# A linear attention chained to two gated networks: each head's 64x64 state in two quarters of the TensorE array

## What is computed

```python
def _attn_ref(q, k, v):
    q_s = exp(q - max(q, axis=-1)); q_s = q_s / (sum(q_s, axis=-1) + 1e-09)
    k_s = exp(k - max(k, axis=2));  k_s = k_s / (sum(k_s, axis=2) + 1e-09)
    kv = np.einsum('bhsd,bhse->bhde', k_s, v)            # a 64 x 64 state for each head
    return np.einsum('bhsd,bhde->bhse', q_s, kv)
x = attn_out.transpose(0, 2, 1, 3).reshape(B * S, H * D)  # 4608 tokens x 512
h = x @ w_in; r = maximum(h, 0); x = (r * r) @ w_out      # 512 -> 2048 -> 512
xn = x / sqrt(mean(x * x) + 1e-06) * rms_g
g = xn @ w_gate; y = (g * sigmoid(g) * (xn @ w_val)) @ w_out2  # 512 -> 1536 -> 512
```

## Time and profile before

| what | us |
| --- | --- |
| median of 3 runs | 1665.97 |
| lowest and highest of them | 1665.57, 1666.49 |
| profiled execution | 1665.29 |
| its span, from the first instruction to the last | 1663.5 |
| PE busy in the span | 1643.8 |

### The profile page before, as it was taken

How to read it: one execution, slowest core, us unless ns; L and a number is a source line. 1 busy time by engine, 2 the same in 40 slices (tenths; PEclk the granted TensorE clock), 3 DMA queues, 4 the chain that set the end, 5 groups by cost and what they waited for, 6 DMA issues and landing times.

```text
span 1663.5 us, 27042 instructions
## 1 busy us (share of the span) xinstructions
PE 1643.8 (99%) x10246; PEld 1496.7 (90%) x10246; DVE 1156.9 (70%) x1749; ACT 616.7 (37%) x1056; POOL 595.7 (36%) x470
## 2 busy tenths in 40 slices
PE   7999999999999999999999999999999998999999
PEld 6999999999988888888888989988988988999999
DVE  6687667666667778888766565546556568877775
ACT  5544334433323333333333333333333344334332
POOL 3554324332002225432237644555555552000000
PEclk9999999999999999999999999999999999999999
DMA  7675545554552353344342323232331244434441
GB/s 262 201 242 182 176 157 191 182 170 145 202 176 89 120 173 120 119 123 125 118 142 70 109 88 134 70 134 75 108 102 63 99 143 163 145 121 149 153 137 54
DMA packets 151745, 230.10 MB, mean 138 GB/s; under 512 B 11840, under 2 KB 75840, under 8 KB 151616
## 3 DMA queue, kind: packets, MB, share of 16 engines
q1 hardware_dynamic: 151616, 228.38, 41.5%
HBM read 143.39 MB, written 84.93 MB: 137 GB/s over the span
## 4 chain that ended last, share of the span: by engine, by line
PE 93%; POOL 2%; DVE 2%; issue 1%; ACT 1%; DMA 0%; SPq 0%; DVEq 0%; POOLq 0%; ACTq 0%
PE bank L1819 16%; PE bank L1820 16%; PE bank L1821 16%; PE bank L1905 7%; PE bank L1906 7%; PE bank L1907 7%; PE bank L1995 5%; PE bank L1996 5%; PE bank L1997 5%; PE bank L1812 2%; PE bank L1792 1%; PE bank L1808 1%; PE bank L1840 1%; PE bank L1841 1%; PE bank L1842 1%
## 5 line engine op out<-in xcount | busy, mean ns | idle before, releaser
L1819 PE MATMUL bank<-TR,SW 128*128 128x512 f32 (+1 forms) x840 | 308.5, 367 | 0.3 <-DVE TR L1554 0.3
L1821 PE MATMUL bank<-TR,SW 128*128 128x512 f32 (+1 forms) x840 | 308.7, 368 | 0.0
L1820 PE MATMUL bank<-TR,SW 128*128 128x512 f32 (+1 forms) x840 | 308.6, 367 | 0.0
L1819 PE MATMUL bank<-TAR,SA 128*128 128x288 f32 x784 | 249.1, 318 | 0.1
L1820 PE MATMUL bank<-TAR,SA 128*128 128x288 f32 x784 | 231.2, 295 | 0.0
L1821 PE MATMUL bank<-TAR,SA 128*128 128x288 f32 x784 | 230.4, 294 | 0.0
L1905 PE MATMUL bank<-GH,W 128*128 128x512 f32 x576 | 224.2, 389 | 0.4 <-DVE GH L1459 0.4
L1906 PE MATMUL bank<-GH,W 128*128 128x512 f32 x576 | 224.2, 389 | 0.0
L1907 PE MATMUL bank<-GH,W 128*128 128x512 f32 x576 | 224.2, 389 | 0.0
L1145 ACT ACTIVATE GH<-g 128x512 fp32r<-128x512 f32 x144 | 91.1, 634 | 241.6 <-DVE g L1454 161.6
L1995 PE MATMUL bank<-SW,OA 128*128 128x256 f32 x630 | 179.0, 284 | 0.0
(11 more groups left out here) (176 smaller groups left out, 3309.4 us busy)
## 6 DMA issues: line engine op xcount, KB each, us to landing
h_scratch<-hb SPq DMA_DIRECT2D x128, 288.0 KB, 2.6
hst<-h_scratch SPq DMA_DIRECT2D x144, 256.0 KB, 2.7
araw<-a_scratch SPq DMA_DIRECT2D x18, 1536.0 KB, 6.8
a_scratch<-group SPq DMA_DIRECT2D x72, 256.0 KB, 2.0
xst<-xn_scratch SPq DMA_DIRECT2D x10, 1024.0 KB, 5.1
xn_scratch<-x SPq DMA_DIRECT2D x9, 1024.0 KB, 5.4
a_scratch<-group SPq DMA_DIRECT2D x48, 192.0 KB, 1.9
out<-ost SPq DMA_DIRECT2D x36, 256.0 KB, 2.1
```

Source lines behind the costliest of these rows:

```text
L1819: nc.tensor.matmul(ps[:, 0:w], w_hi[:, cc], x_hi[:, c], start=opens and c == 0, stop=False, skip_group_check=True)
L1820: nc.tensor.matmul(ps[:, 0:w], w_lo[:, cc], x_hi[:, c], start=False, stop=False, skip_group_check=True)
L1821: last = nc.tensor.matmul(ps[:, 0:w], w_hi[:, cc], x_lo[:, c], start=False, stop=c == 1, skip_group_check=True)
```

## The change

In batches 1 to 7 X0 and X1 no longer split the tokens but the heads. X0 is head 0 (rows 0 to 63 of the array), X1 is head 1 (rows 64 to 127). Each is two matmuls with the same 64x64 weights, one diagonal quarter of `bd`: the first on tokens 0 to 287 with its result in partitions 0 to 63 of the bank (columns 0 to 63 of the array), the second on tokens 288 to 575 with its result in partitions 64 to 127. So the four matmuls of a unit lie in four different quarters of the array. Both rounds now wait for Q1, and both stand at offset 6. ACT reads each bank with two copies of 64 partitions and 288 columns, four in a unit where there were two of 128 partitions; all four stand at offset 7. Batch 0 keeps its form.

```diff
-UNIT_PE = [("KM", -3), ("Q0", 0), ("Q1", 1), ("KV", 2), ("X0", 6), ("X1", 7)]
+UNIT_PE = [("KM", -3), ("Q0", 0), ("Q1", 1), ("KV", 2), ("X0", 6), ("X1", 6)]
-UNIT_ACT = [("qexp", -7), ("kexp", -1), ("readQ0", 1), ("readQ1", 2), ("readX0", 7), ("readX1", 8)]
+UNIT_ACT = [("qexp", -7), ("kexp", -1), ("readQ0", 1), ("readQ1", 2), ("readX0", 7), ("readX1", 7)]
...
-                    if b:
+                    if b == 0:
+                        nc.scalar.activation(xa[:, c, half * TA:(half + 1) * TA], ps[:, 0:TA], ACT.Copy).then_inc(taken_act, 1)
+                    else:
                         act.wait_ge(ta_lo, split_a(b - 1, B22))
-                    nc.scalar.activation(xa[:, c, half * TA:(half + 1) * TA], ps[:, 0:TA], ACT.Copy).then_inc(taken_act, 1)
+                        for t in range(2):
+                            last = nc.scalar.activation(xa[half * D:(half + 1) * D, c, t * TA:(t + 1) * TA],
+                                                        ps[t * D:(t + 1) * D, 0:TA], ACT.Copy)
+                        last.then_inc(taken_act, 1)
...
-                    wait_taken(act, ROUND_NO[b, "X1" if i in (B12, B22) else "X0", 1 if i in (B11, B12) else 3] - 1)
+                    wait_taken(act, ROUND_NO[b, "X1" if i in (B12, B22) or b else "X0", 1 if i in (B11, B12) else 3] - 1)
...
-                    wait_taken(pe, ROUND_NO[b, "Q1" if half else "Q0", c] - 1)
-                    last = nc.tensor.matmul(ps[:, 0:TA], m.bd, m.qT[:, half * TA:(half + 1) * TA], start=True, stop=True)
+                    wait_taken(pe, ROUND_NO[b, "Q1" if half or b else "Q0", c] - 1)
+                    if b == 0:
+                        last = nc.tensor.matmul(ps[:, 0:TA], m.bd, m.qT[:, half * TA:(half + 1) * TA], start=True, stop=True)
+                    else:
+                        head = slice(half * D, (half + 1) * D)
+                        for t in range(2):
+                            last = nc.tensor.matmul(ps[t * D:(t + 1) * D, 0:TA], m.bd[head, head],
+                                                    m.qT[head, t * TA:(t + 1) * TA], start=True, stop=True)
```

## The result

The changed kernel takes 1676.4 us (1675.99 to 1678.43, four runs), the kernel before 1665.77 us beside it. The medians lie 10.6 us apart, where +8.4 was forecast. The ratio is 1.0068, with an interval from 1.0057 to 1.008 (9.5 to 13.3 us), so it is slower beyond the noise, by well under 2%. In the profiled executions the span went from 1663.5 to 1674.7 us, +11.2.

The account below looks back on a forecast made before the run. TensorE was taken to bound the kernel. Six times 0.73, 0.44 and 0.45 us for held KM, less 10 x 0.13 saved, gave +8.4 us: 1665.97 + 8.4 = 1674.4 us, range 1668.8 to 1685.5.

Parts of the forecast that it names:

- TensorE sets the end, and every wait in the later batches is paid in full: Later batches: TensorE busy 359.53 of 360.00 us, so each microsecond X takes from it and each new wait counts fully.
- step 14: Place met six times where KM waits for ACT's copies of X0; forecast +0.73 us each, some 0.86 us of it wait.
- Four quarters at once cost 0.835 us of TensorE: X rounds of a unit: 0.485 us streaming plus 0.35 way in and out, against 0.97; 0.13 us saved in 28 units.
- A copy of 64x288 takes the 0.41 us of one of 128x288: ACT's reads of X: a copy's time goes by its columns, so half the partitions still take 0.41 us.
- The next copy follows 0.30 us after the start: ACT's two copies of an X bank start 0.30 us apart, so the bank is free 0.30 us later.
- The rest is unchanged: Outside the X rounds and KM's waits nothing moves; the stage ends about 8 us later.
- Which KM wait, and why: KM waits for ACT's X0 copies 18 times, some 0.8 us at six places and 0.5 us at twelve, nowhere else.
- Heads in turn: Rival for the X rounds: only column halves run at once, head 1 waits for head 0; +19.0 us, 1685.0; chance 0.13.
- Strict program order: Rival for the X rounds: no record passes another, so quarters overlap by one record; +25.8 us, 1691.8; chance 0.03.
- A free switch: Rival: going into and out of quarters costs nothing, X takes 0.485 us; -0.1 us, 1665.9; chance 0.05.
- Short reads: Rival for ACT's copies: 0.26 us behind 0.15, every held KM 0.30 us sooner; +3.0 us, 1669.0; chance 0.07.
- The wait holds KM alone: Rival: filler matmuls for other banks pass the waiting KM, so waits cost nothing; -3.6 us, 1662.4; chance 0.06.

Follow-up runs that it names:

- the single copies: Changed kernel, but ACT reads each X bank with one copy of 128x288 (data lands in the wrong half); 1668.84 us, ratio 1.0022 to the kernel before.
- the heads one step apart: Changed kernel with X1 back at offset 7 and its reads at 8, so each visit to the quarters holds one head; 1684.26 us, single run.
- the order alone: Kernel before, whole X rounds and one copy each, with X1 moved to offset 6 and its read to 7; 1669.78 us, ratio 1.0026.
- the kernels with Q0's read ahead: KM, its read and the exponential one step later, Q0's read before the exponential: changed kernel 1664.4 us, kernel before 1666.71 us; later variants follow.
- the last kernel: Changed kernel, Q0's read before the exponential, KM and unit 1 of later batches one step later, batch 1's KM, readKM, kexp offsets old; 1663.4 us, ratio 0.9987.

## Why the prediction was right, and which sizes it had wrong

- **TensorE sets the end, and every wait in the later batches is paid in full.** Right, and more than in full: in the starts of the filler the 18 holds cost 0.93 us at step 14 and 0.63 elsewhere, some 13 us where 10.2 show as idle, and the 28 cheaper X give back 3.4.
- **Four quarters at once cost 0.835 us of TensorE.** Right to 0.01 us. A unit with no KM behind it, where four rows show what ends and what follows:

```profile
249.92 0.29 PE L1832 MATMUL bank<-TAR,SA 128*128 128x288 f32 x1
250.14 0.72 PE L1822 MATMUL bank<-qT,bd 64*64 64x288 f32 x8
250.79 0.40 PE L1830 MATMUL bank<-TAR,SA 128*128 128x288 f32 x1
251.03 0.30 PE L1831 MATMUL bank<-TAR,SA 128*128 128x288 f32 x1
```

  From the first filler matmul to the third it is 251.03 - 249.92 = 1.11 us, less two spacings of 0.133: 0.84 for X. The 0.35 us read off a KV round for the way in and out is borne out, and the 0.70 us visits of one head say it again.
- **A copy of 64x288 takes the 0.41 us of one of 128x288.** Right: 0.41 (0.407 in the median).
- **The next copy follows 0.30 us after the start.** This is the step that failed in size. It was read off two copies of 128 partitions, and it is 0.42 between the two halves. Each of the 18 held KM is released 0.12 us later for it. Some 0.05 comes back by a smaller error: behind such a wait KM's weight load shows for 0.05 us (its record lasts 0.32 us where an undisturbed one lasts 0.27) and not for the 0.11 of the forecast. So each hold comes out 0.07 us dearer, +1.3 us, and 8.4 + 1.3 = 9.7. The pieces give the same: 6 x 0.80 + 12 x 0.51 - 10 x 0.12 = 4.8 + 6.1 - 1.2 = +9.7.
- **The rest is unchanged.** This fell a little short. The medians differ by 0.9 us more than that, the spans of the two traces by 1.5, and the traces have these 1.5 at the changes of stage behind the attention. TensorE waits there three times for DVE where the kernel before waits once, 0.4 us for `GH`:

```profile
PE bank L1916 <- DVE GH L1464: 0.8, 2, 0.4
...
PE bank L1830 <- DVE group L1624: 0.4, 1, 0.4
...
PE bank L2006 <- DVE SW L1633: 0.2, 1, 0.2
```

  That is 1.0 us more. What ties them to the change isn't shown; the single copies and the heads one step apart have the second wait for `GH` too, the order alone doesn't.
- **Which KM wait, and why.** Right: 18 and nowhere else. In the middle units it is the block product behind X and the ACT copy that waits for it that make the reads late. The order alone (+4.5 us) and the single copies (+3.6 us) each show one part of this: KM is held without the added copy too, and most of the loss goes with it.
- **Heads in turn.** Fell: the second head adds 0.02 us to a visit.
- **Strict program order.** Fell: X's records form two waves, four of them started within 0.04 us, and a visit of two quarters has two records in its first wave. So the second record of a matmul, which needs the quarter of the first, starts behind the first records of the other quarters. The Trainium skill ("TensorE: Matmul & The Clock Gate", Part 3, The mechanism) has matmuls start strictly in program order. The forecast took each record for a matmul of its own and found that KV's trace does not agree; if the two records are one matmul, the trace does not speak against the page, since the first records could be in the order of the program, some 0.01 us apart. No run here tells the two readings apart. By either, the 25.8 us of this rival fell.
- **A free switch.** Fell: 0.84 us, not 0.485.
- **Short reads.** Fell by the 0.41 us copies. (Half of 0.41 is 0.205, so the forecast's low bound of "half of it all", a copy of 0.26 behind 0.15, is not quite that; its end at 1669.0 us would be some 1 us lower.)
- **The wait holds KM alone.** Fell: between the end of X and KM there is no filler record at step 14, though filler for other banks stands right behind KM.

## What to carry to other kernels

Cutting a matmul into parts that run side by side saves stream time only once per visit and pays the change of tile form each time (0.35 us here, against 0.485 saved); gather as much as possible into one visit. Count the readers too: here the same data came out in twice as many instructions, and a copy of half the partitions took as long as one of all, so the buffer came free 0.4 us later and TensorE stood still for it 18 times, which turned a gain of some 2 us into a loss of 10.6. Read such a hold from the starts of the matmuls on both sides and not from the idle time alone. Where a spacing of instructions is carried from one shape to another, look whether the two start at the same partition; and before a round is moved out of a wait, ask whose buffer it will then take and which engine's queue reads that.

## What the runs showed that was not expected

- ACT overlaps a copy with the tail of the one before (0.30 us apart for 0.41 us copies, 0.18 for 0.29), and loses this where the first partition of the input or of the output changes (0.42 and 0.30 apart). A changed bank alone costs nothing that these runs tell apart from that.
- The two records of a float32 matmul don't stay together when others stand in other quarters: four records within 0.04 us, then four more. Two quarters take 0.70 us and four 0.72.
- Stretches of 3.4 us at half the clock go with part of the spread. Of the 27 runs of the kernel before beside the kernels with Q0's read ahead, eight had a mean granted clock of 1.000 and a median of 1664.65 us, twelve 0.999 and 1665.35, seven 0.998 and 1666.95.
- Not tried: columns of its own for KM in another bank, and half of the copies on DVE, which is idle for 103.86 of 360 us there in the last kernel.
